# An attention kernel with two mixture-of-experts layers: rows doubled on chip in the opening, row adds in halves, another order at the seam

## The reference

```python
# q, k, v: (2, 8, 768, 64): 16 heads; centroids: (8, 16, 64)
q_assign = argmax(unit(q) @ unit(c).T); k_assign = argmax(unit(k) @ unit(c).T)
scores = where(q_assign[:, None] == k_assign[None, :], q @ k.T / 8, -1e9)
attn = softmax(scores) @ v                       # -> x: (1536, 512)
# routed layer: each token goes to one of 8 experts
logits = unit(x) @ unit(expert_emb).T / tau      # expert_emb: (8, 512)
e = argmax(logits); x = softmax(logits)[e] * (relu(x @ w1[e]) @ w2[e])
# dense layer: every token goes through all 8 experts
P = exp(x @ w_gate - max); eight rounds: P /= P.sum(1); P /= P.sum(0); P *= N / E
out = sum over e of P[:, e:e+1] * (relu(x @ W1[e]) @ W2[e])
```

## Time and profile before

| | |
|---|---|
| median of 3 runs | 1591.67 us (1590.71 to 1593.67) |
| the profiled execution's own time | 1594.29 us |
| its span, first to last instruction | 1592.5 us |
| TensorE busy | 1568.3 us, 98% |
| VectorE busy | 1190.0 us, 75% |
| ScalarE busy | 770.6 us, 48% |
| GpSimd busy | 263.7 us, 17% |
| mean granted TensorE clock | 0.995 |

### The profile page before, as it was taken

One profiled execution on the slowest core, in us unless ns is written; L12 is line 12 of the kernel. 1 busy time (PEld: TensorE's weight loads), 2 busy tenths in 40 slices (PEclk: granted clock), 3 DMA queues, 4 the chain that ended last, 5 costly groups with the idle time before them and its releaser, 6 DMA issues.

```text
span 1592.5 us, 27473 instructions
## 1 busy us (share of the span) xinstructions
PE 1568.3 (98%) x8404; PEld 1390.7 (87%) x8404; DVE 1190.0 (75%) x2026; ACT 770.6 (48%) x1418; POOL 263.7 (17%) x343
## 2 busy tenths in 40 slices
PE   8999999999999999999999999999999999999998
PEld 7999999778888788989999898989899998989897
DVE  7999999999999976876656666666656566666664
ACT  5777779888888852323232323233232333232321
POOL 2111111342333550000100100010001001100102
PEclk9999999999999999999999999999999999999999
DMA  4222323354344310100110010011001100100002
GB/s 101 61 60 69 79 59 90 86 198 148 143 151 151 106 41 27 40 28 27 47 33 27 29 51 27 27 40 40 27 27 45 35 27 28 52 26 27 27 0 79
DMA packets 123701, 94.92 MB, mean 60 GB/s; under 512 B 66345, under 2 KB 101161, under 8 KB 123633
## 3 DMA queue, kind: packets, MB, share of 16 engines
q1 hardware_dynamic: 120848, 86.01, 17.8%
q0 software_dynamic: 2480, 8.13, 1.5%
q10 hardware_dynamic: 304, 0.05, 0.0%
HBM read 87.88 MB, written 6.29 MB: 59 GB/s over the span
## 4 chain that ended last, share of the span: by engine, by line
PE 88%; DVE 7%; issue 3%; ACT 2%; DVEq 0%; DMA 0%; ACTq 0%; POOL 0%
PE moe_bank L1381 11%; PE moe_bank L1383 11%; PE moe_bank L1382 11%; PE moe_bank L1356 10%; PE moe_bank L1359 10%; PE moe_bank L1358 10%; PE attn_ps_out L447 3%; PE attn_ps_probs_t L428 2%; PE moe_bank L1316 2%; PE moe_bank L1318 2%; PE moe_bank L1317 2%; PE moe_bank L1299 2%; PE moe_bank L1301 2%; PE moe_bank L1300 2%; DVE attn_scores L697 1%
## 5 line engine op out<-in xcount | busy, mean ns | idle before, releaser
L2035 DVE SCALAR_TENSOR_TENSOR all_x<-moe_bank,all_x 128x512 f32<-128x512 f32 x336 | 251.4, 749 | 130.8 <-PE moe_bank L1383 130.2
L1356 PE MATMUL moe_bank<-moe_x_t_hi,all_w_hi 128*128 128x384 f32 x896 | 303.0, 338 | 2.0 <-DVE all_w_lo L889 1.4
L1359 PE MATMUL moe_bank<-moe_x_t_hi,all_w_lo 128*128 128x384 f32 x896 | 302.5, 338 | 0.0
L1381 PE MATMUL moe_bank<-moe_w_hi,moe_h_hi 128*128 128x512 f32 x768 | 302.3, 394 | 0.0
L1358 PE MATMUL moe_bank<-moe_x_t_lo,all_w_hi 128*128 128x384 f32 x896 | 301.1, 336 | 0.0
L1382 PE MATMUL moe_bank<-moe_w_lo,moe_h_hi 128*128 128x512 f32 x768 | 300.5, 391 | 0.0
L1383 PE MATMUL moe_bank<-moe_w_hi,moe_h_lo 128*128 128x512 f32 x672 | 264.5, 394 | 0.0
L1356 PEld LDWEIGHTS moe_bank<-moe_x_t_hi,all_w_hi 128*128 128x128 f32 x896 | 168.4, 188 | 13.4 <-issue 2.0
L1358 PEld LDWEIGHTS moe_bank<-moe_x_t_lo,all_w_hi 128*128 128x128 f32 x896 | 168.4, 188 | 10.0
L1359 PEld LDWEIGHTS moe_bank<-moe_x_t_hi,all_w_lo 128*128 128x128 f32 x896 | 168.2, 188 | 0.0
L2196 POOL TENSOR_TENSOR moe_w_sums<-moe_dense_w_raw 128x256 f32<-128x256 f32 x32 | 24.8, 774 | 842.4 <-DVE all_w_lo L889 842.4
(11 more groups left out here) (339 smaller groups left out, 3071.4 us busy)
## 6 DMA issues: line engine op xcount, KB each, us to landing
all_w_raw<-in_moe_w SPq DMA_DIRECT2D x8, 2048.0 KB, 7.5
moe_w_raw<-in_moe_w SPq DMA_DIRECT2D x8, 2048.0 KB, 8.3
moe_dense_w_raw<-in_moe_w SPq DMA_DIRECT2D x64, 256.0 KB, 2.9
moe_dense_w_raw<-in_moe_w SPq DMA_DIRECT2D x32, 512.0 KB, 3.4
attn_q_raw<-in_q SPq DMA_DIRECT2D x32, 192.0 KB, 3.0
attn_k_raw<-in_k SPq DMA_DIRECT2D x32, 192.0 KB, 3.5
attn_v_raw<-in_v SPq DMA_DIRECT2D x16, 192.0 KB, 3.5
tokens<-all_x SPq DMA_DIRECT2D x32, 96.0 KB, 1.9
```

The lines of the kernel that those rows point to most:

```text
L1356: pe.matmul(out, hi[:, s, k, :], XH[chunk][:, x, k, :], start=(start and k == 0), stop=False, skip_group_check=True)
L1359: mm = pe.matmul(out, lo[:, s, k, :], XH[chunk][:, x, k, :], start=False, stop=(stop and k == 1), skip_group_check=True)
L1381: pe.matmul(out, HH[h][hidden][:, rows], W2H[j][:, f, :], start=(f == 0), stop=False)
L2035: dve.scalar_tensor_tensor(acc, y, PROB[:, row, bass.ds(at, 1)], acc, ALU.mult, ALU.add).then_inc(y_added, 1)
```

## The change

- **Opening.** Head 0's and head 1's q and k are loaded once each and copied into the second half of their tile on chip: q of head 0 by VectorE, k of head 0 by ScalarE, q and k of head 1 by GpSimd. `UnitRows` becomes one chain per array. The centroids' chain stays on VectorE and comes first; the embeddings are loaded by SP, squared and summed and written by ScalarE, with their Newton steps on VectorE later. The similarities of head 0 start tile by tile. Key ids come ahead of eight of head 1's transposes, and the masks and maxima of the first two tiles are interleaved with head 1's low parts. The third tile's scores come ahead of head 1's similarities and the experts' transposes. `WARM` has six entries in place of three.
- **Items.** In loop n GpSimd gathers item n+2 and then adds item n-1, in two halves of 256 columns; the first half waits until VectorE has done w2 parts 0 and 1 of the next item, the second until it has done parts 2 and 3. In item 0's tile w2's part 1 moves ahead of the gates' sum.
- **Seam.** All token sums are GpSimd's. The weight sums (0,1) come ahead of the last add and of pair 5's token sums. ScalarE's high parts of these weight sums come right behind the first product's copy, VectorE's low parts of them ahead of the first unit's corrections. In `last_tile` VectorE's low part of the first hidden half comes ahead of w2 parts 2 and 3. TensorE transposes pair 5 one product earlier.

```diff
-WARM = (8, 4, 6)
+WARM = (7, 4, 2, 3, 4, 6)
 # UnitRows: one object per array
+        cents = UnitRows(mem, "centroids", ...)
+        embeddings = UnitRows(mem, "embeddings", expert_emb, ...)
+    def sums_of_squares(self, act):
+        act.wait_ge(self.loaded, 16)
+        act.activation(self.square[:], self.raw[:], ACT.Square, accum_out=self.s[0]).then_inc(self.summed, 1)
+    def write_by_scalar(self, act):
+        act.wait_ge(self.step, self.SCALED)
+        for out, raw in self.outputs():
+            act.activation(out, raw, ACT.Copy, scale=self.s[2]).then_inc(self.written, 1)
 # SP
-            for half in range(2):
-                sp.dma_start(QR[0][:, :, half, :], ...).then_inc(first_q, 16)
-            for half in range(2):
-                sp.dma_start(KR[0][:, :, half, :], ...).then_inc(first_k, 16)
+            sp.dma_start(QR[0][:, :, 0, :], ...).then_inc(first_q, 16)
+            sp.dma_start(KR[0][:, :, 0, :], ...).then_inc(first_k, 16)
             sp.dma_start(VR[0][:], ...).then_inc(first_v, 16)
-            load(1, 1)
+            embeddings.load(sp)
+            sp.dma_start(QR[1][:, :, 0, :], ...).then_inc(second_q, 16)
+            sp.dma_start(KR[1][:, :, 0, :], ...).then_inc(second_k, 16)
+            sp.dma_start(VR[1][:], ...).then_inc(raw_loaded[1], 16)
+            sp.dma_start(TAU[:, 0:1], ...).then_inc(tau_loaded, 16)
 # TensorE
-            pe.wait_ge(prep_lo, 3)
-            similarities(0, 0, ps_o[:, P:P + 2 * T * NC], 0)
-            similarities(0, 0, ps_o[:, P:P + 2 * T * NC], T).then_inc(prep_ready, 1)
+            for first in range(0, 2 * T, 4):
+                pe.wait_ge(prep_lo, first // 4 + 1)
+                mm = similarities(0, 0, ps_o[:, P:P + 2 * T * NC], first, 4)
+            mm.then_inc(prep_ready, 1)
+            scores(0, 0, 0)
             pe.wait_ge(raw_loaded[1], LOADS)
             transpose_raw(1, 0, 4, ps_s[1][:, 0]).then_inc(prep_ready, 1)
-            transpose_raw(1, 4, 4, ps_s[1][:, 1]).then_inc(prep_ready, 1)
-            transpose_raw(1, 8, 4, ps_t[:, 1]).then_inc(prep_ready, 1)
-            scores(0, 0, 0)
+            warm(WARM[2], ps_s[1][:, 1])
             pe.wait_ge(idb_ready, 1)
             key_ids(ps_t[:, 0], 0)
             key_ids(ps_p[:], 3)
+            transpose_raw(1, 4, 4, ps_s[1][:, 1]).then_inc(prep_ready, 1)
+            transpose_raw(1, 8, 4, ps_t[:, 1]).then_inc(prep_ready, 1)
             pe.wait_ge(prep_lo, 5)
             scores(1, 1, 0)
+            warm(WARM[3], ps_o[:])
+            pe.wait_ge(max_done, 1)
+            scores(2, 2, 0)
+            warm(WARM[4], ps_o[:])
             pe.wait_ge(kid_ready, 2)
             pe.wait_ge(prep_lo, 6)
             similarities(1, 1, ps_p[:], 0)
...
-            pe.wait_ge(max_done, 1)
-            scores(2, 2, 0)
 # ScalarE
+            act.wait_ge(first_k, 16)
+            act.activation(KR[0][:, :, 1, :], KR[0][:, :, 0, :], ACT.Copy).then_inc(first_k2, 1)
             prep(0, 0, 0)
             prep(0, 0, 1, ps_t[:, 0])
-            prep(0, 0, 2, ps_t[:, 1])
             act.activation(CH[:], ...); act.activation(CHL[:], ...)
+            prep(0, 0, 2, ps_t[:, 1])
+            embeddings.sums_of_squares(act)
+            embeddings.roots(act)
+            act.activation(TABLE[:], c["rank16"][:, 0:1], ACT.Exp)
+            embeddings.write_by_scalar(act)
 # VectorE
+            cents.sums(dve)
+            dve.wait_ge(first_q, 16)
+            dve.tensor_copy(QR[0][:, :, 1, :], QR[0][:, :, 0, :]).then_inc(first_q2, 1)
+            cents.scale(dve)
+            cents.write(dve)
             prep(0, 0, 0)
-            prep(0, 0, 1, ps_t[:, 0])
-            prep(0, 0, 2, ps_t[:, 1])
             low(CL[:], ...); low(CHL[DH:P, :], ...)
+            prep(0, 0, 1, ps_t[:, 0])
+            prep(0, 0, 2, ps_t[:, 1])
+            embeddings.scale(dve)
...
-            prep(1, 1, 1, ps_s[1][:, 1])
-            prep(1, 1, 2, ps_t[:, 1])
-            rows.write(dve, 1)
             mask(0, 0, 0)
             maxima(0, 0)
+            prep(1, 1, 1, ps_s[1][:, 1])
             mask(1, 1, 0)
             maxima(1, 1)
+            prep(1, 1, 2, ps_t[:, 1])
             mask(2, 2, 0)
 # GpSimd
+            for raw, loaded in ((QR[1], second_q), (KR[1], second_k)):
+                pool.wait_ge(loaded, 16)
+                pool.tensor_copy(raw[:, :, 1, :], raw[:, :, 0, :]).then_inc(raw_loaded[1], 32)
 # GpSimd, add_rows(n)
-                pool.tensor_tensor(OUT[t], OUTZ[s], Y[n % 2][:], ALU.add).then_inc(ry_added, 1)
+                for half, (cols, done) in enumerate(((slice(0, D // 2), ry_half), (slice(D // 2, D), ry_added))):
+                    if n + 1 < ITEMS:
+                        pool.wait_ge(rw2_lo, W2_PARTS * (n + 1) + 2 * half + 2)
+                    if half == 1:
+                        pool.wait_ge(ry_half, n + 1)
+                    pool.tensor_tensor(OUT[t, cols], OUTZ[s, cols], Y[n % 2][:, cols], ALU.add).then_inc(done, 1)
 # GpSimd, loop over n: gather(n + 2), then
-                add_rows(n)
-                if n >= ITEMS - 5 and n < ITEMS - 3:
-                    all_token_sums(n - (ITEMS - 5))
+                else:
+                    add_rows(n - 1)
+                if ITEMS - 4 <= n < ITEMS - 2:
+                    token_sums(n - (ITEMS - 4))
+            add_rows(ITEMS - 3)
             add_rows(ITEMS - 2)
             next_weight_sums()
-            all_token_sums(2); all_token_sums(3); all_token_sums(4)
+            for p in range(2, 5):
+                token_sums(p)
+            weight_sums(0, 1)
             add_rows(ITEMS - 1)
             token_sums(5)
-            weight_sums(0, 1)
 # TensorE, first_unit
+                transpose_pair(5)
                 pe.wait_ge(copied, 3)
                 multiply(a, 0, 0, A22, T4, False, True).then_inc(chain, 1)
-                transpose_pair(5)
 # ScalarE, first_unit
                 act.activation(CP1[:], a, ACT.Copy).then_inc(copied, 1)
+                summed_weights(0, 1)
                 hi_parts(3)
...
                 hi_parts(5)
-                summed_weights(0, 1)
 # VectorE, last_tile
+                h_part(n, 0)
                 w2_part(n, r, 2)
                 w2_part(n, r, 3)
-                h_part(n, 0)
 # VectorE, first_unit
                 lo_parts(3)
-                token_sums(5)
                 lo_parts(4)
-                low(0, hh, hl, Q11, CP1[:], 1)
...
                 dve.tensor_tensor(CU3[:], b, CU3[:], ALU.add).then_inc(summed, 1)
+                summed_weights(0, 1)
+                low(0, hh, hl, Q11, CP1[:], 1)
                 low(0, hh, hl, Q22, CU3[:], 2)
                 low(0, hh, hl, Q21, a, 3)
                 lo_parts(5)
-                summed_weights(0, 1)
```

More of the change, by code:

```diff
@@ L143, in load, with __init__ @@
-    def load(self, act):
-        for j, (rows, _) in enumerate(self.arrays):
-            act.dma_start(self.raw[j][:], rows).then_inc(self.loaded[j], 16)
+    SCALED = 6
+    def __init__(self, mem, name, rows, outs):
+        self.rows, self.outs = rows, outs
+        self.raw = mem.sbuf(f"{name}_raw", list(rows.shape))
+        self.square = mem.sbuf(f"{name}_square", list(rows.shape))
+        self.norms = mem.sbuf(f"{name}_norms", [P, 4])
+        self.s = [self.norms[0:rows.shape[0], j:j + 1] for j in range(4)]
+        self.loaded, self.squared, self.summed = [mem.sem(f"{name}_{what}") for what in ("loaded", "squared", "summed")]
+        self.root, self.step, self.written = [mem.sem(f"{name}_{what}") for what in ("root", "step", "written")]
@@ L160, in scale @@
-        dve.wait_ge(self.root, 1)
-        newton(dve, step, self.SUMS, s[:, 0, :], s[:, 1, :], s[:, 2, :], s[:, 3, :])
-        dve.wait_ge(step, self.SUMS + 6)
-    def write(self, dve, j):
-        rows, outs = self.arrays[j]
-        for out in outs:
-            raw = self.raw[j][:].rearrange("r (h d) -> r h d", d=DH) if len(out.shape) == 3 else self.raw[j][:]
-            dve.tensor_scalar(out, raw, self.s[0:rows.shape[0], 2, j:j + 1], None, ALU.mult).then_inc(self.step, 1)
+        dve.wait_ge(self.root, 1)
@@ L361, in transpose_sims, with similarities @@
                 mm.then_inc(prep_ready, 1)
-            def similarities(g, j, out, first):
+            def similarities(g, j, out, first, n=T):
                 cols = bass.ds((g % H) * NC, NC)
-                for m in range(first, first + T):
+                for m in range(first, first + n):
                     sims = out[:, m * NC:(m + 1) * NC]
@@ L522, in tensor @@
             similarities(1, 1, ps_p[:], 0)
-            pe.wait_ge(rows.step, rows.DONE)
+            pe.wait_ge(embeddings.written, 2)
             for h in range(H):
```

104 lines of the change are left out of this document (44 added, 60 removed).

## The result

The changed kernel takes 1598.46 us in the median (eight runs, 1595.85 to 1600.67), the kernel before, beside it, 1591.61. That is 6.9 us slower by the medians; the ratio as estimated from the runs is 1.0033, interval 1.0025 to 1.0042, so 4.0 to 6.7 us, and in the later sets of 11 to 28 runs the kernel before has medians of 1592.4 to 1593.2. For the time 1590.4 was forecast, 1594.5 was the upper end. The profiled execution, the longest of the eight, took 1600.67 us of its own time; its span is 1598.9, 6.4 more than before's.

What follows compares the result with a forecast made beforehand. From 582.84 us TensorE works 1002.84 of 1009.66 us, so only opening, loop and seam could change: -1.6 - 0.5 + 0.8 = -1.3 us, median 1591.67 to 1590.4 us, range 1586.4 to 1594.5.

Steps and rivals of the forecast that it cites:

- Opening, -1.6 forecast: Opening, up to VectorE's first step: maxima start at 21.2 instead of 23.44, 2.2 sooner, of which 1.6 us was taken.
- All at full clock they take 2.5: Opening: head 0's 24 similarities on TensorE run at 2.4 GHz, from 8.1 to 10.6 us, a gain of 4.1.
- rival C: Opening: TensorE's clock falls behind the similarities, the 1.6 is gone; no change, 1592.0 us; chance 0.22.
- the delay of up to 0.3: Opening: VectorE's copy starts up to 0.3 us later by ports shared with GpSimd; the opening would then save 1.3.
- Items, -0.5 forecast: Loop over the 19 items: the first of three TensorE waits, 0.5 us, goes; an ordinary item gains nothing.
- the bound of -1.4: Loop: the most the items could gain, 1.4 us, which is all of TensorE's three waits there.
- the three waits: Loop: TensorE waits for the hidden rows' low part, 0.5 us at most each; one goes, two only move later.
- Seam, +0.8 forecast (-1.1 to +2.8): Last item to second unit: unit 1's second product starts at 583.6 instead of 582.84; bounds no collision, two more.
- rival B: Seam: ScalarE's early wait for weight sums (0,1) sets the pace, eight collisions; total +4.7, 1596.4 us; chance 0.10.
- I let two collide: 572: Seam: two of GpSimd's 21 operations meet VectorE subtractions, so its sums end at 572 instead of 569.9 us.
- the first unit starts only some 1.0 sooner, near 566.2: Seam: with the 1.9 us wait gone, TensorE next waits for token tiles' low parts, startable at 555.5 instead of 556.4.
- Behind the seam: From 582.84 us to the end: no line of the change runs there, so the stretch keeps its length.

Runs made afterwards that it cites:

- h1: Changed kernel with VectorE's low part of the last hidden rows set back behind the last two w2 subtractions; 1.0032 of the kernel before.
- e1: Kernel before with the change's opening alone; 1.0018 of the kernel before.
- f3: Changed kernel with TensorE turning the embeddings ahead of head 1's similarities instead of behind them; 1.0032 of the kernel before.
- f1: Changed kernel with the second unit's weight sums (0,1) late again on GpSimd, ScalarE and VectorE; 1.0024 of the kernel before.
- f6: Kernel before with the items' part, and VectorE's low part of the last hidden rows ahead of the last two w2 subtractions; 1.0010 of the kernel before.
- e4: Changed kernel with ScalarE and VectorE splitting weight sums (0,1) behind pair 5's parts again, GpSimd's order left; 1.0035 of the kernel before.

## Why the prediction was wrong

**Opening, -1.6 forecast, +0.9 and +1.0 found.** The order of events was right: at full clock the mask starts at 13.8 to 13.9 (13.7 forecast) and the step's maxima at 21.9 (21.2), worth 1.0 at head 2 against before's profile. What failed is the step "All at full clock they take 2.5", and rival C's price for its opposite. C said that a fall costs the 1.6 and no more; it costs 2.9 (head 2 at -1.0 against +1.9), and all of that ahead of the first mask: with the fall the ids start 1.5 later (12.22 against 10.73 in h1) and the mask another 1.3 behind them, since similarities, scores, transposes, padding and key ids all stand one behind the other on TensorE. From the mask to the step's maxima both take 8.1, and VectorE's wait of 1.80 at the fold is there at either clock (h1's line):

```profile
21.52 0.29 DVE L806 TENSOR_SCALAR all_fold<-attn_ps_out,attn_tau 128x64 f32<-128x64 f32 x1 [1.80 <-PE attn_ps_out L542]
```

My sum also set a full clock against one profile of before with a long fall (6.6 us), and so booked the clock as the change's gain. I also let the fall come only behind the similarities; in e1 it came behind TensorE's own wait of 2.3 us for the second scores, which stands in my working as VectorE's time and not as TensorE's idleness. The heads' +1.0 I did not foresee at all; no row of before shows it.

The two sentences that rested on pages: the copy on VectorE took 0.44 (0.36 in e1 and h1), within the bounds, though GpSimd was building constants beside it, so of the delay of up to 0.3 that I estimated by the Trainium skill (SBUF — State Buffer, "Who interferes with whom") at most 0.1 shows. In the loop the same rule holds: a pair of subtractions takes 2.35 with GpSimd out of the way and took 3.47 beside its add. And that the clock follows what TensorE lately did (the Trainium skill, TensorE: Matmul & The Clock Gate, "What's actually happening") agrees with the falls behind the waits, 2.3 us in e1 and 4.2 in h1.

**Items, -0.5 forecast, -1.3 found**, near the bound of -1.4. I let two of the three waits merely move; all three went.

**Seam, +0.8 forecast (-1.1 to +2.8), +4.0 found.** The mechanism, the price of the early sums, was in the sum and in rival B; the sizes were wrong. Taken back by the 1.6 us that the changed kernel was late at the last item, the gated half started at 555.8 (555.4 forecast) and the sums ended at 574.1 (572 forecast). The step that failed is "I let two collide: 572": four operations met subtractions and took 1.18 to 1.73, 3.0 us in all where I had 2.0; start and small waits make the other 1. So pair 3's high parts started at 575.1, not 573.0. The chain from there was right: where the clock held behind the wait, the seam is +2.7 to +2.8, the forecast's 0.8 and these 2.0. The rest of the +4.0 is the clock, which I let recover: falls behind the wait cost 1.0 in f3 and 2.0 in the changed kernel, 0.4 in the mean of seven, and the profile of before that I measured against has a fall of its own (0.71 from 555 to 560 us), which makes its seam 1.2 longer than the two others' and the mean of the three 0.8 shorter. In all ten profiles with GpSimd's early sums some stretch of five microseconds at the seam stands at 0.52 to 0.78; of the nine without, six show none below 1.00.

Another step was wrong too: "the first unit starts only some 1.0 sooner, near 566.2". It started at 569.16, less the 1.6 at 567.6, and before at 567.26, 0.3 later instead of 1.0 sooner. VectorE's wait of 0.85 for ScalarE and pair 2's token sums, ready at 565.4 (563.8 less the 1.6) for 560.6 before, took it; I costed GpSimd's chain only at its end. Under the early sums this cost next to nothing, since ScalarE waited for GpSimd anyway; it is what f1 and f6 still pay.

**Behind the seam** nothing changed its length, as forecast.

## What to carry to other kernels

When work moves from one engine's queue to another's, walk the receiving queue from its first operation to each of its readers, not only to the last one: here the weight sums were late for ScalarE in its new place, and with ScalarE set back it was the last add, queued behind them, that was late (e4). If two waits overlap, undo both before calling either harmless (the two pieces cost 4.5 and 1.5 alone, and 4.3 together, not 6). In a stretch as short as an opening, price before and after at either clock level, and let the whole chain on TensorE run at the lower one; the gain forecast was 1.6, the difference between the levels 2.9.

## What the runs showed that I had not expected

Identical openings differ by 2.6 us (before) and 2.9 us (changed) between executions, with the moment at which TensorE's clock falls and how long it stays low; one profile says little about a stretch of 40 us. And a loop whose instructions are all the same ran 0.6 and 0.8 us faster over thirteen heads when four and eight memsets were put far ahead of it, once each; with four, 0.5 came back before item 0.
